# Attention, expert layer and feed-forward on one core: feed-forward tokens reordered by expert, router logits issued later

## Chip, cores and metric

The kernel runs on one core of a Trainium2 chip. The metric is device time in microseconds (us) of one execution; lower is better. The text calls the engines PE (TensorE; PEld is its weight load), DVE (VectorE), ACT (ScalarE), POOL (GpSimd) and SP (SyncE, which issues DMAs only). An engine works through its own instructions in order; semaphores order the engines among each other.

## What is computed

```python
def reference(q, k, v, proj, w_gate, w_noise, noise, w1, w2, w_in, w_out):
    # attention: 2 batches x 8 heads, 768 tokens, head size 64, masked to equal hash buckets
    mask = bucket(q @ proj)[:, :, :, None] == bucket(k @ proj)[:, :, None, :]
    x = softmax(where(mask, q @ k.T / 8, -1e9)) @ v         # as (1536 tokens, 512)
    # 8 experts, each 512 -> 1024 -> 512; the two with the largest noisy logits per token
    noisy = x @ w_gate + log1p(exp(x @ w_noise)) * noise
    top2, weight = two_largest(noisy), softmax_of_the_two
    for e in range(8):
        y[mask_e] += weight_e * (relu(x[mask_e] @ w1[e]) @ w2[e])
    # feed-forward 512 -> 2048 -> 512
    h = y @ w_in
    return (h * sigmoid(1.702 * h)) @ w_out
```

## The kernel before

Every large product is made of three passes of TensorE over 32-bit numbers that are split in a rounded ("high") part and a rest ("low" part): high x high, high x low, low x high. So each weight chunk of 128 x 1024 numbers (512 KB) passes through four hands: SP loads it into one of two buffers `staged` (`stage_chunk`, L381; chunk n is loaded only when the low part of chunk n-2 is done), ACT or POOL rounds it into the weight buffer W (`high_w` on ACT, L1292; on POOL L478), and POOL subtracts to get the low part (L480, in `split_chunk`). W holds two blocks of 8 chunks: an even and an odd one. Blocks 0 to 7 are the experts (chunks 0 to 3 are w1, 4 to 7 are w2), block 8 (`E`) is w_in, block 9 (`E + 1`) is w_out. The list `order` says in which order chunks are loaded. ACT rounds the chunks of experts 1 to 7 itself; those of blocks 0, 8 and 9 are rounded by POOL.

The stages, one after the other:

- **Attention**, to 301 us.
- **Router**, from 302 us. For each of 12 token blocks T of 128 tokens, PE transposes four pieces (L708) into one of three PSUM banks (`router_bank`), ACT takes the high part (L1256), DVE the low part (L996). After each three blocks (a group) PE computes their logits (`router_logits`, L699); ACT copies them out (L1260, L1263) and PE transposes them (L716). DVE then finds the two largest, and works out with matmuls against `one` and `tri` (L722, L723) which slot each token takes in each expert's tile of 416 rows (L1048 to L1068). Two sets of 24 small matmuls (L727, L731) turn that into the gather lists `gather_i` (L1096 and L1100).
- **Experts.** Tiles t = 0 to 7, one expert each; tiles 8 to 14 exist for experts with over 416 tokens, and none is used with these inputs. POOL gathers a tile's tokens with four indirect DMAs (`gather_x`, L521). In `expert_tile`, each of 8 steps f has PE's `hidden_up(t, f + 1)` (12 matmuls, L763) and `hidden_down(t, f)` (12 matmuls, L781), then transposes of the tile before (`transpose_y`, L794) and of the tile after (`transpose_x`, L742). ACT and DVE split the hidden values (L1285 and L1111), and the step f of tile t also has ACT's `high_w(t + 1, f)`. `rows_y` copies the finished rows and ACT sends them to `ys_dram` (L1311), with a second copy to tiles 8 to 14 (L1313), so that these hold finite numbers.
- **Feed-forward.** 12 token blocks in four groups of three. For each block POOL gathers two rows per token from `ys_dram` (`gather_y`, L579; it first waits until all rows of all used tiles have landed), ACT weights the one (`scale_x2`, L1356), DVE adds the other (`add_x2`, L1168), PE transposes (L848), and ACT and DVE split (L1360, L1172). Then in 16 steps f per group: `up(g, f + 1)` (12 matmuls, L861), sigmoid and products on ACT and DVE (L1366, L1179, L1369, L1182), `down(f)` (9 matmuls, L876). The input of the next group is made inside the steps named in `PREP = (4, 8, 12)`: scaled at f - 3, added at f - 2, transposed and split at f. A loop runs groups 0 to 2; group 3 stands alone. After each group ACT and DVE copy the outputs (L1387, L1197) and SP stores them with one DMA (L444).

## Time and profile before

| | us |
|---|---|
| median of 3 runs (lowest, highest) | 979.61 (979.21, 980.17) |
| the profiled execution | 978.34 |
| its span, first to last instruction | 976.6 |
| PE busy in the span | 884.1 (91%) |
| POOL busy | 315.0 (32%) |
| DVE, ACT busy | 402.6, 402.8 (41% each) |
| chain that ended last, PE's share | 82% |
| mean granted clock of TensorE | 0.962 of full |

Times in all rows are us from the span's start. A windows row gives, for a stretch, its length, the busy time of PE, PEld, DVE, ACT and POOL with the number of instructions, the granted clock, the DMA engines' share and GB/s.

### The profile page before, as it was taken

How to read it: one execution, taken by the hardware profiler on the slowest of the kernel's cores; microseconds unless marked ns; L12 is line 12 of the kernel's file. 1: busy time of each engine (PE TensorE's matmuls, PEld its weight loads, DVE VectorE, ACT ScalarE, POOL GpSimd, SP SyncE). 2: the span in 40 equal slices, each digit the busy share in tenths (PEclk: the TensorE clock that was granted, in tenths of full speed). 3: DMA queues.
4: the chain of work that ended last, by engine and by line, in shares of the span. 5: the costliest groups of instructions: out<-in, count | busy, mean ns of one | idle time of the engine just before them, and what ended most of it. 6: DMA issues, size and time to landing. Idle time of an engine off the chain costs nothing.

```text
span 976.6 us, 13334 instructions
## 1 busy us (share of the span) xinstructions
PE 884.1 (91%) x4910; PEld 770.6 (79%) x4910; DVE 402.6 (41%) x746; ACT 402.8 (41%) x687; POOL 315.0 (32%) x199
## 2 busy tenths in 40 slices
PE   3799999999997399999999999994699999999997
PEld 3566676676664289999999999994598999999996
DVE  4577776676864612222222222211443333333222
ACT  1566676667573223343443444411233323332222
POOL 1222020000330035655655646697971010000000
PEclk8799999999999679999999999997799999999999
DMA  7445633652323023556556555464421010000000
GB/s 164 111 116 147 168 73 95 168 125 63 93 87 109 1 74 110 190 155 184 178 159 183 166 171 173 149 200 156 140 87 44 32 43 21 32 0 0 33 1 33
DMA packets 66778, 103.34 MB, mean 106 GB/s; under 512 B 31676, under 2 KB 33724, under 8 KB 66716
## 3 DMA queue, kind: packets, MB, share of 16 engines
q1 hardware_dynamic: 55216, 76.65, 28.3%
q0 software_dynamic: 4480, 13.11, 4.5%
q10 hardware_dynamic: 7020, 12.78, 3.6%
q8 instruction: 36, 0.59, 0.2%
q14 instruction: 26, 0.21, 0.1%
HBM read 64.57 MB, written 19.07 MB: 86 GB/s over the span
## 4 chain that ended last, share of the span: by engine, by line
PE 82%; DVE 7%; ACT 3%; issue 3%; DMA 2%; SPq 2%; POOL 1%; ACTq 0%; DVEq 0%; POOLq 0%
PE psS L763 15%; PE psS L861 14%; PE psS L876 9%; PE psS L781 7%; PE psV L656 6%; PE psT L642 5%; PE psS L631 5%; PE psV L876 5%; PE psV L781 4%; PE psM L781 4%; DVE W L930 2%; PE psM L618 2%; PE psT L794 1%; ACT probT L1232 1%; PE psM L613 1%
## 5 line engine op out<-in xcount | busy, mean ns | idle before, releaser
L480 POOL TENSOR_TENSOR W<-staged,W 128x1024 fp32r<-128x1024 f32 x80 | 191.9, 2401 | 120.8 <-ACT W L1292 116.1
L763 PE MATMUL psS<-xT_hi,W 128*128 128x416 f32 x512 | 144.0, 363 | 0.8 <-DVE xT_lo L1105 0.8
L861 PE MATMUL psS<-x2T_hi,W 128*128 (+1 forms) x512 | 133.7, 342 | 1.6 <-DVE x2T_lo L1172 1.6
L1223 ACT ACTIVATE prob<-psS,exp_arg 128x768 f32<-128x768 f32 x96 | 95.5, 995 | 38.2 <-DVE exp_arg L939 38.0
L936 DVE TENSOR_REDUCE neg_max<-psS 128x1 f32<-128x768 f32 x96 | 91.5, 953 | 45.6 <-PE psS L631 44.8
L631 PE MATMUL psS<-W 128*128 128x384 f32 x384 | 93.9, 368 | 11.7 <-DMA W<-k_hi 9.6
L1232 ACT ACTIVATE probT<-psT 128x768 f32<-128x768 f32 x96 | 78.1, 813 | 57.8 <-PE psT L642 56.4
L1111 DVE SCALAR_TENSOR_TENSOR hT_lo<-psS,hT_hi 128x416 fp32r<-128x416 f32 x64 | 37.9, 592 | 152.6 <-ACT hT_hi L1285 144.2
L861 PEld LDWEIGHTS psS<-x2T_hi,W 128*128 128x128 f32 x512 | 94.2, 190 | 6.8 <-issue 2.0
L763 PEld LDWEIGHTS psS<-xT_hi,W 128*128 128x128 f32 x512 | 94.2, 191 | 2.3 <-issue 1.1
L631 PEld LDWEIGHTS psS<-W 128*128 128x128 f32 x384 | 65.1, 194 | 39.1 <-issue 34.4
L1179 DVE TENSOR_TENSOR g_sb<-psS,sig 128x384 f32<-128x384 f32 x64 | 35.7, 558 | 138.3 <-ACT sig L1366 138.3
L1366 ACT ACTIVATE sig<-psS 128x384 f32<-128x384 f32 x64 | 31.5, 492 | 144.6 <-PE psS L861 144.6
L763 PE MATMUL psS<-xT_lo,W 128*128 128x416 f32 x256 | 91.0, 355 | 0.0
L478 POOL TENSOR_TENSOR W<-staged,ones_col 128x1024 fp32r<-128x1024 f32 x24 | 45.8, 1910 | 134.8 <-DMA staged<-in_moe_w 96.3
L861 PE MATMUL psS<-x2T_lo,W 128*128 (+1 forms) x256 | 86.9, 340 | 0.0
L642 PE MATMUL psT<-ident,prob 128*128 128x128 f32 x576 | 80.7, 277 | 5.4 <-ACT probT L1232 5.3
L876 PE MATMUL psS<-W,g_hi 128*128 128x512 f32 x256 | 79.9, 393 | 2.9 <-issue 2.9
L642 PEld LDWEIGHTS psT<-ident,prob 128*128 128x128 f32 x576 | 67.3, 142 | 16.2 <-issue 12.7
L1292 ACT ACTIVATE W<-staged 128x1024 fp32r<-128x1024 f32 x56 | 59.1, 1055 | 30.7 <-DVE x_sb L1126 17.2
L781 PE MATMUL psS<-hT_hi,W 128*128 128x416 f32 x256 | 69.5, 353 | 0.0
L656 PE MATMUL psV<-probT,v_raw 128*64 128x384 f32 x360 | 68.0, 499 | 0.0
(215 smaller groups left out, 1375.5 us busy)
## 6 DMA issues: line engine op xcount, KB each, us to landing
staged<-in_moe_w SPq DMA_DIRECT2D x64, 512.0 KB
ys_dram<-x_sb ACTq DMA_DIRECT2D x60, 208.0 KB
W<-q_hi SPq DMA_DIRECT2D x32, 192.0 KB, 3.4
W<-k_hi SPq DMA_DIRECT2D x32, 192.0 KB, 3.7
staged<-in_moe_w_in SPq DMA_DIRECT2D x8, 512.0 KB
staged<-in_moe_w_out SPq DMA_DIRECT2D x8, 512.0 KB
q_raw<-in_q SPq DMA_DIRECT2D x16, 192.0 KB, 4.0
k_raw<-in_k SPq DMA_DIRECT2D x16, 192.0 KB, 3.7
```

The costliest lines, as they stand in the source:

```text
L480: nc.gpsimd.tensor_tensor(W[:, at + BLOCK:at + BLOCK + CH], staged[:, n % 2], W[:, at:at + CH].bitcast(F32), ALU.subtract).then_inc(s_spli ...
L631: last = nc.tensor.matmul(psS[:, n % 2, half, 0:HALF], stack(slot, a)[:, qt * P:(qt + 1) * P], stack(slot, b_)[:, half * HALF:(half + 1) * ...
L642: last = nc.tensor.transpose(psT[:, half, j * P:(j + 1) * P], prob[:, n % 2, c * P:(c + 1) * P], ident[:])
L656: last = nc.tensor.matmul(av_bank(hd)[half * D:(half + 1) * D, 0:HALF], v_raw[:, hd // 2 % 2, hd % 2, c * D:(c + 1) * D], probT[:, hd % 2, ...
L763: mm = nc.tensor.matmul(psS[:, 0, f % 2, 0:TM], W[:, at:at + P], x[:, t % 2, c], start=c == 0 and n == 0, stop=c == DC - 1 and n == 2)
L781: mm = nc.tensor.matmul(y_bank[d][:, 0:TM], W[:, at:at + P], h[:, f % 2], start=f == 0 and n == 0, stop=f == FC - 1 and n == 2)
L861: mm = nc.tensor.matmul(psS[:, 0, f % 2, 0:GN], W[:, at:at + P], x[:, bass.ds(buf + c * GN, GN)], start=c == 0 and n == 0, stop=c == DC - ...
L876: mm = nc.tensor.matmul(out_bank[j], gp[:, f % 2, j * P:(j + 1) * P], W[:, at:at + DM], start=f == 0 and n == 0, stop=f == GC - 1 and n == 2)
L936: nc.vector.tensor_reduce(neg_max[:, o, 0:1], psS[:, o, :, 0:HALF], mybir.AxisListType.XY, ALU.max, negate=True).then_inc(s_stat, 1)
L1223: nc.scalar.activation(prob[:, o, :].rearrange("p (a c) -> p a c", a=2), psS[:, o, :, 0:HALF], ACT.Exp, bias=exp_arg[:, o, 0:1], scale=exp ...
L1232: nc.scalar.activation(probT[:, hd % 2, :, t * P:(t + 1) * P].rearrange("p (a c) q -> p a c q", a=2), psT[:, :, 0:HALF].rearrange("p a (c ...
L1292: A(W[:, at:at + CH], staged[:, n % 2], ACT.Copy).then_inc(s_whi, 1)
```

## The change

Three parts.

1. Router: four banks instead of three; the logits of group g are issued after the transposes of group g + 1, so after blocks 5, 8 and 11, and once more at the end; ACT copies them after blocks 6, 9 and 11.
2. The order of tokens in the feed-forward. A second ranking (`mine`, `sofar`, `order_f`) sorts tokens by the larger of their two experts. Per token a record of 8 words (two slots, token number, two weights) is written to its sorted place in `rec_dram` by 12 indirect DMAs on POOL, placed ahead of the weight chunks of tile 2, behind four register loads of `needs` (how many tiles' rows each group of 384 tokens needs). SP reads the records back behind chunk (3, 7). The gathers then go by records, and the outputs are scattered to their token numbers by indirect DMAs on POOL, three per group, in place of SP's store.
3. The seam between experts and feed-forward. Group 0 is gathered, weighted and added by POOL (`first_x2`) between weight chunks, while PE is in expert 7; PE transposes it right behind expert 7 into three free banks. The chunks of w_in and w_out are loaded and split in a mixed order, w_out is rounded by ACT (`high_w(E + 1, ...)` in group 0), PE waits for halves of w_in, and `PREP` moves to (6, 10, 14). Group 0 stands outside the loop. The tiles' second copies are spread over other tiles (`filled_by`), and also go to tiles 6 and 7.

```diff
-        PREP = (4, 8, 12)
+        PREP = (6, 10, 14)
+        def filled_by(t):
+            return ((E - 2, E - 1, E), (E + 1, E + 2), (E + 3, E + 4), range(E + 5, TILES))[t] if t < 4 else ()
+        def first_bank(j):
+            return (psM, psV, psS[:, 1, 1])[j]
-        order = [(b, c) for b in range(E + 2) for c in range(8)]
+        order = [(b, c) for b in range(E) for c in range(8)]
+        order += [(E, 4), (E, 6), (E, 0), (E, 2), (E + 1, 0), (E + 1, 1), (E, 1), (E + 1, 2), (E, 3), (E, 5)]
+        order += [(E + 1, 3), (E, 7), (E + 1, 4), (E + 1, 5), (E + 1, 6), (E + 1, 7)]
...
# SP
             for block, c in order[8:8 * E]:
                 stage_chunk(block, c)
+                if (block, c) == (3, 7):
+                    sp.wait_ge(s_recs, 16 * TT)
+                    sp.dma_start(rec_s[:], rec_dram.rearrange("(t p) r -> p t r", p=P)).then_inc(s_rec, 16)
...
# POOL
-                if block in (0, E, E + 1):
+                if block in (0, E):
...
             for t in range(2, E):
                 gather_x(t)
+                if t == 2:
+                    pool.wait_ge(s_class, 1)
+                    need = [pool.value_load(needs[0:1, g:g + 1], min_val=1, max_val=TILES) for g in range(GROUPS)]
+                    for T in range(TT):
+                        nc.gpsimd.indirect_dma_start(out=rec_dram[:, :], out_offset=bass.IndirectOffsetOnAxis(ap=pos_i[:, T:T + 1].bitcast(U32), axis=0),
+                                                     in_=rec[:, T], in_offset=None).then_inc(s_recs, 16)
                 for c in range(8):
                     release(t - 2, c)
                     split_chunk(t, c)
...
             def gather_y(T):
+                j = T % GT
                 if T == 0:
-                    pool.wait_ge(s_fill, 16 * JB * (TILES - E))
-                    pool.wait_ge(s_ys, used * (16 * JB) + LEAD)
+                    pool.wait_ge(s_rec, 16)
+                    pool.wait_ge(s_fill, 16 * JB * (TILES - E + 2))
+                    pool.wait_ge(s_xT, DC * E)
+                if j == 0:
+                    pool.wait_ge(s_ys, need[T // GT] * (16 * JB) + LEAD)
...
+            def first_x2(j):
+                pool.wait_ge(s_yg[j][0], 16)
+                pool.wait_ge(s_yg[j][1], 16)
+                nc.gpsimd.tensor_tensor(yg[:, j], yg[:, j], rec_f[:, 8 * j + 3:8 * j + 5, None].to_broadcast([P, 2, DM]), ALU.mult).then_inc(s_x2a, 1)
+                pool.wait_ge(s_x2a, LEAD + j + 1)
+                nc.gpsimd.tensor_tensor(yg[:, j, 1], yg[:, j, 0], yg[:, j, 1], ALU.add).then_inc(s_x2, 1)
+            def scatter_out(g):
+                for j, (s, n) in enumerate(((s_oa, 2 * g + 1), (s_od, g + 1), (s_oa, 2 * g + 2))):
+                    pool.wait_ge(s, LEAD + n)
+                    T = GT * g + j
+                    nc.gpsimd.indirect_dma_start(out=out[:, :], out_offset=bass.IndirectOffsetOnAxis(ap=rec_s[:, T, 2:3].bitcast(U32), axis=0),
+                                                 in_=out_sb[:, j], in_offset=None).then_inc(s_out, 16)
+            split_next(E, 4)
+            split_next(E, 6)
+            for j in range(GT):
+                gather_y(j)
+            split_next(E, 0)
+            for j in range(GT):
+                first_x2(j)
+            split_next(E, 2)
+            split_next(E + 1, 0)
+            split_next(E + 1, 1)
+            for j, cs in enumerate((((E, 1), (E + 1, 2)), ((E, 3), (E, 5)), ((E + 1, 3), (E, 7)))):
+                gather_y(GT + j)
+                for bc in cs:
+                    split_next(*bc)
+            for c in range(4, 8):
+                split_next(E + 1, c)
+            for g in range(GROUPS):
+                for j in range(GT):
+                    if g + 2 < GROUPS:
+                        gather_y(GT * (g + 2) + j)
+                scatter_out(g)
...
# PE, router
-                if T >= 3:
-                    pe.wait_ge(s_rod, T - 2)
+                if T >= 4:
+                    pe.wait_ge(s_rod, T - 3)
-                if T and T % GT == 0:
+                if T >= 2 * GT - 1 and T % GT == GT - 1:
                     router_logits(T // GT - 1)
+            pe.wait_ge(s_mine, 1)
+            flat = mine[:].rearrange("p e t -> p (e t)")
+            nc.tensor.matmul(psT[:, 1, 0:TT * E], one[:], flat, start=True, stop=True)
+            nc.tensor.matmul(psT[:, 1, 256:256 + TT * E], tri[:], flat, start=True, stop=True).then_inc(s_mrank, 1)
# PE, feed-forward
                 if f % GC == 0:
+                    pe.wait_ge(s_split, split_by(E, 2))
+                if f == GC // 2:
+                    pe.wait_ge(s_split, split_by(E, 7))
...
-                    pe.wait_ge(s_split, LEAD + 8 * (E + 1) + f // 2 + 1)
+                    pe.wait_ge(s_split, split_by(E + 1, f // 2))
...
# ACT, feed-forward
+                    if first_group and f % 2 == 0 and f + 2 < GC:
+                        high_w(E + 1, f // 2 + 1)
...
+            for j in range(GT):
+                high_x2(0, j, j, True)
+            high_w(E + 1, 0)
             hidden(0, 0)
+            group(0, False, True)
```

DVE: three gate operations move from ahead of the slots' chain to its end, two (`larger`, `mine`) come ahead of it, the cast to `slot_i` goes, and sixteen small ones (the three gate operations among them) (`sofar`, `order_f`, `pos_f`, `pos_i`, `reached`, `need_f`, `needs`, `rec`) stand between the lists for the spare tiles and the cast of L1100.

## Rows read from the trace of the kernel before

**Rows 1.** Windows: an expert stretch, the seam, a feed-forward stretch.

```profile
400.00:440.00 40.00, 40.00 (x228) 39.25 (x227) 9.58 (x16) 15.94 (x25) 22.89 (x12) 1.00 0.55 168
667.60:693.50 25.90, 5.30 (x29) 3.87 (x29) 9.75 (x10) 5.97 (x10) 19.08 (x14) 0.61 0.53 164
704.00:757.00 53.00, 53.00 (x272) 47.97 (x271) 19.67 (x29) 15.80 (x30) 26.01 (x17) 1.00 0.22 74
```

**Rows 2.** Chain that ended last, in the router: start, length, what.

```profile
305.32 1.54 PE psS L699 x8
306.86 0.45 PE psT L708 x4
...
308.81 0.70 DVE xTg_lo L996
...
318.35 1.54 PE psS L699 x8
```

**Rows 3.** The same chain, end of the routing.

```profile
331.67 0.19 DVE slot_c L1065
...
341.47 4.35 PE psM L731 x24
...
346.04 0.90 issue
```

**Rows 4.** Timeline of POOL, tile 1's last chunk to tile 2's first.

```profile
395.92 1.00 POOL L521 DMA_INDIRECT x_sb<-x_dram,gather_i  x1 [0.18 <-issue]
...
399.80 0.99 POOL L521 DMA_INDIRECT x_sb<-x_dram,gather_i  x1 [0.30 <-issue]
401.63 2.38 POOL L480 TENSOR_TENSOR W<-staged,W 128x1024 fp32r<-128x1024 f32 x1 [0.84 <-PE psS L763]
```

**Rows 5.** Timeline of ACT in tile 1, step f = 2 and the next.

```profile
410.64 1.05 ACT L1292 ACTIVATE W<-staged 128x1024 fp32r<-128x1024 f32 x1
411.59 0.51 ACT L1285 ACTIVATE hT_hi<-psS 128x416 fp32r<-128x416 f32 x1
```

**Rows 6.** Chain: PE begins hidden_down(1, 4).

```profile
416.76 1.14 PE psS L781 x6
```

**Rows 7.** Timeline of SP: one load of a weight chunk issued.

```profile
638.41 0.33 SPq L381 DMA_DIRECT2D staged<-in_moe_w_in  x1
```

**Rows 8.** Timeline of POOL: that chunk waited for, and a later one rounded.

```profile
643.08 1.90 POOL L478 TENSOR_TENSOR W<-staged,ones_col 128x1024 fp32r<-128x1024 f32 x1 [0.38 <-DMA staged<-in_moe_w_in]
...
651.73 1.89 POOL L478 TENSOR_TENSOR W<-staged,ones_col 128x1024 fp32r<-128x1024 f32 x1
```

**Rows 9.** Chain across the seam between experts and feed-forward.

```profile
667.06 0.58 PE psM L781 x3
...
681.80 3.67 DMA yg<-ys_dram,slot_i
...
693.52 6.06 PE psS L861 x24
699.58 2.63 issue
...
704.57 2.11 PE psS L861 x12
```

**Rows 10.** Timeline of ACT: the last rows of tile 7 sent off.

```profile
671.72 1.00 ACTq L1311 DMA_DIRECT2D ys_dram<-x_sb  x2
```

**Rows 11.** Timeline of DVE: one low half of g, one of the next group's input.

```profile
699.18 2.73 DVE L1182 TENSOR_TENSOR g_lo<-g_sb,g_hi 128x384 fp32r<-128x384 f32 x1 [0.59 <-ACT g_hi L1369]
...
739.97 0.69 DVE L1172 TENSOR_TENSOR x2T_lo<-psT,x2T_hi 128x512 f32 x1 [1.14 <-ACT x2T_hi L1360]
```

**Rows 12.** Timeline of POOL beside the first of these.

```profile
699.16 2.35 POOL L480 TENSOR_TENSOR W<-staged,W 128x1024 fp32r<-128x1024 f32 x1
```

**Rows 13.** Chain: the transposes ahead of the second of these.

```profile
738.65 0.44 PE psT L848 x4
```

**Rows 14.** Timeline of SP: the last store.

```profile
972.94 0.33 SPq L444 DMA_DIRECT2D out<-out_sb  x1
```

More of the change, by code:

```diff
@@ L439, in _ @@
                 stage_chunk(block, c)
-            for g in range(GROUPS):
-                sp.wait_ge(s_oa, LEAD + 2 * g + 2)
-                sp.wait_ge(s_od, LEAD + g + 1)
-                half = GROUPS // B
-                sp.dma_start(out_rows[g // half, :, g % half * GT:(g % half + 1) * GT, :], out_sb[:]).then_inc(s_out, 16)
             sp.wait_ge(s_x, 16 * B)
-            sp.wait_ge(s_out, LEAD + 16 * GROUPS)
+            sp.wait_ge(s_out, 16 * TT)
         @block.gpsimd
         def _(pool):
+            nc.gpsimd.memset(rec[:].bitcast(F32), 0.0)
             nc.gpsimd.memset(ident[:], 0.0).then_inc(s_const, 1)
@@ L583, in _ @@
-            for T in range(3):
-                gather_y(T)
-            for c in range(1, 8):
-                release(E - 1, c)
-                split_chunk(E + 1, c)
-                if c % 2 and 3 + c // 2 < 6:
-                    gather_y(3 + c // 2)
-            for T in range(6, TT):
-                gather_y(T)
+                    nc.gpsimd.indirect_dma_start(out=yg[:, j, k_], out_offset=None, in_=ys_dram[:, :],
+                                                 in_offset=bass.IndirectOffsetOnAxis(ap=rec_s[:, T, k_:k_ + 1].bitcast(U32), axis=0)
+                                                 ).then_inc(s_yg[j][k_], 16)
```

167 lines of the change are left out of this document (102 added, 65 removed).

## The prediction

> **What bounds the kernel now.** I read the page first, then windows by stage, then the chain of waits at each place that the change touches. In an expert stretch PE is busy for all of the 40 us at the full clock, and POOL for 22.9; in the first feed-forward group PE is again full, 53 of 53 us, with POOL at 26.0 [rows 1]. In these stages time is lost only if somebody makes PE wait. The seam between them is different: 25.9 us with 5.3 us of PE work at a mean clock of 0.61 [rows 1]. The chain there runs from PE's last matmul (ends 667.64) over the landing of tile 7's rows, the gathers and the first weighted blocks to PE's first `up` at 693.52 [rows 9]. The router is a second place: its logits come every 4.34 us (three periods from 305.32 to 318.35), while the PE work in a period is 1.57 + 3 x 0.45 = 2.9; PE waits for DVE's low halves [rows 2]. ACT, DVE and POOL are at or under 41% elsewhere, but their order matters: each is a queue, and PE's next operand may stand behind a wait of another's.
>
> **Router.** Four banks and later logits let transposes 3 to 5 run before the first logits, which can still start at 305.3. From there PE has 1.54 + 1.35 per group. The last logits then need the twelfth low half; at the pace of 0.6 to 0.7 us a piece [rows 2], behind ACT, I get 313.1 in place of 318.35: **-5.2** (PE's work alone would give 312.7, -5.6; if ACT's copies delay the last pieces, -4.5). The sixteen small DVE operations at about 0.2 us [rows 3], a few of them 0.3, make some 3.8 us. They run beside 24 matmuls of 4.35 us, after which comes the cast that PE waits for: nothing; without that cover up to 1. The two operations ahead of the slots take the place of three.
>
> **Tile 1: POOL comes late.** Before, POOL issues the last gather for tile 2 at 399.80 and takes the low part of chunk (2, 0) at 401.63, without a pause [rows 4]. Now four register loads and twelve indirect DMAs stand between. Each DMA costs a pitch of 1.29 (395.92 to 399.80 are three) [rows 4]; that is for gathers of 104 rows, and scatters of 32 bytes a row are not in this trace. Twelve make 15.2. For a register load the nearest row is PE's: 0.90 us from `gather_i` to its first matmul [rows 3], of which 0.14 is the usual gap, so 0.76 each, 3.0 together. So POOL is free at 400.8 + 3.0 + 15.2 = 419.0, and (2, 0) is split at 421.5. Only then may SP load chunk (2, 2). A load that was waited for took 643.08 - 638.41 = 4.67 [rows 7, 8], so it lands at 426.2. ACT has that rounding as its work at 410.64 [rows 5] and is an in-order queue: behind it stands the rounding of hT for `hidden_down(1, 4)`. 1.05 + 0.51 on ACT, 0.59 on DVE and gaps put it at 428.6, where PE began at 416.76 [rows 6]: 11.8 lost. After it each second chunk has a cycle of load 4.67, rounding 1.05, low part 2.38 and gaps, 8.4 us, against 9 to 10 of PE, so the queue recovers slowly; working it through gives two more waits of 1.0 and 1.4, and PE restarts at the lower clock (1.2 GHz; 24 matmuls took 6.06 in place of 2 x 2.11 [rows 9]), of which about 0.5 is not covered by these. **+14.5.** Lower bound 0: if the block took under 6.1 us, the rounding would come within the 3.4 us of slack that hT has (`down` and `up` of 2.3 each, less 1.2 for ACT and DVE). Upper bound +18, at 1.3 us per load and 1.4 per DMA. ACT's extra copies of tile 0's rows (two more issues per step) fit in that slack: nothing, at most 1. SP's reading of the records sits behind chunk (3, 7), whose follower is wanted 9 us later: nothing, at most 3.
>
> **Seam.** POOL has done (7, 7) at 633.9. Then: four splits of w_in at 4.3, the step that rows 8 show twice over (643.08 to 651.73), six gathers at 1.26, and three times a multiply of 1.9 and an add of half of 2.4: 17.3 + 7.6 + 9.6 = 34.5, so 668.4. Bounds for `first_x2`, which the trace doesn't show: 2.6 to 6 us each; the ends are 667 and 677. PE has group 0's transposes done at 671.9. ACT is bound by the sending of tile 7's rows to 672.72 [rows 10]; three roundings at a pitch of 0.5 and a DVE low half of 0.69 bring PE's first `up` to 675.2 in place of 693.52: **-18.3**. Before, the first `down` came 8.7 us behind it: slow clock 1.84, and a `g_lo` of 2.73 us where others take 0.56. That one is put down as 2.63 of "issue" [rows 9], but it ran from 699.18 beside a POOL subtract of 699.16 to 701.51 and ended 0.4 behind it [rows 11, 12]. With POOL idle there it is 4.6; PE pauses for only 3.3 us now, and whether the clock falls in that, as it did in the 25.9 us (mean 0.61 [rows 1]), no row decides; I take half: **-3.2** (-4.1 or -2.3).
>
> **Group 0: POOL is the bound.** PE could start `up(0, 8)` at 675.2 + 8 x 2.11 + 7 x 2.10 + 0.8 = 707.5. It needs (E, 7). POOL can't start on (E + 1, 1) before ACT has rounded it, behind `hidden(0, 1)`: 682.2. Then in its queue: low part 2.4, two gathers 2.5, split 4.3, 2.4, 2.5, two splits 8.7, 2.5, 2.4, split 4.3, and gaps: 715. So 7.2 lost, of which PE stands 5 at `down(6)`. To this comes what rows 11 and 12 show: DVE's SBUF-with-SBUF subtract is held to the end of a POOL operation, then holds POOL for 0.4. Six such meetings in POOL's chain add 2.5: **+9.7** (5 to 13). The Trainium skill ("SBUF — State Buffer", section "SBUF: two separate sides") says that DVE and GpSimd take one shared pair of ports as an exclusive lock for a whole instruction; the trace agrees (2.73 for 0.56), and by it `hidden`'s other operations, with PSUM on one side, stay untouched, as do those of expert 7.
>
> **PREP (6, 10, 14).** The last block of the next group is now transposed at f = 14, and the next thing that PE does is `up(g + 1, 0)`, which needs its low half. That came at 740.66, 1.57 behind PE's transposes (738.65 + 0.44) [rows 11, 13]. Before, one more step covered it. Three group changes at 1.6: **+4.8** (3.9 to 5.4).
>
> **Tail.** SP's one store, issued at 972.94 [rows 14], becomes three scatters, the first from 972.5, the third from 975.1. Landing 3.67 behind its issue, as a gather [rows 9], it ends at 978.7 against 976.6: **+2.1** (0.5 to 4). By the Trainium skill ("DMA: Bandwidth & Descriptors", section "Anatomy of one DMA — SWDGE (gpsimd) path"), 2.0 us and 0.6 for 256 KB, this term would be 1.1, an estimate; the rows are longer, and I go by them.
>
> **Sum.** -5.2 - 18.3 - 3.2 + 14.5 + 9.7 + 4.8 + 2.1 = +4.4. The profiled execution has 978.34 for a span of 976.6 and would have 982.7. It lies 1.3 under the median of 979.61, so I forecast **984.0**.
>
> **Rivals.**
> 1. *POOL's record writes are cheap.* If a 32-byte scatter costs about what a direct DMA costs ACT (0.3 to 0.5 us) and the loads little, the block stays at or near 6 us and PE doesn't stop in tile 1: 984.0 - 14.5 = 969.5, faster. It decides at 6.1 us for the whole block; at 12 us the time would be 976. For it: the data are small. Against: the issue of a gather looks like a fixed cost. Chance 0.2.
> 2. *They are dearer.* The same block at 25 to 30 us, because twelve in a row wait for room: 994. For it: PE then also meets the low clock twice. Against: six gathers in a row kept their pitch. Chance 0.1.
> 3. *The first group isn't ready at the seam.* `first_x2` at 6 us each or gathers later than I have them put (E, 2) behind 675.2, by 2 to 5 us: 988. POOL was busy all through expert 7 already. Chance 0.1.
> 4. *Group 0 isn't starved*: ACT and POOL interleave better than my chain, 5 us less: 979, no change. Chance 0.1.
>
> **Numbers.** Forecast as worked out 0.5, own range 978 to 990. About 0.2% (2 us) is what a measurement can tell from no change. Slower by more: 0.5 x 0.75 + 0.1 + 0.1 + a little of the fourth = 0.58. Faster by more: rival 1's 0.2, a share of the others, 0.26. Within: 0.16. The range takes in most of rivals 1 and 2: 971 to 993.
>
> **What the profile would show.** Right: a PE gap of some 12 us in tile 1 with ACT's L1292 waiting for a load; logits 2.9 us apart; the first `up` about 8 us behind the last `down` of tile 7; PE waiting at f = 6 and 8 of group 0 for POOL's low parts; three waits of 1.6 at the group changes. Wrong: POOL done with its record writes before about 407; no wait at f = 8; a seam over 12 us.

## The result and the profile after

The changed kernel takes **990.25 us** (median of 4 runs, 989.34 to 991.05) against 979.89 for the kernel before (4 runs, 979.21 to 981.80): ratio 1.0102, 95% interval 1.0084 to 1.0121. That is 1.0% slower, in the direction of the forecast of 984.0 and inside its range of 971 to 993, though just outside the 978 to 990 of the case that was worked out; it is slower by 10.4 us where 4.4 were forecast. The profiled execution has 991.04 for a span of 989.3; the one before had 978.34 for 976.6. So 12.7 us of span have to be explained.

Windows of the kernel after: the expert stretch of [rows 1], the seam, the first feed-forward group, the other three; then a short one behind a group change. The columns are those of [rows 1].

```profile
400.00:440.00 40.00, 34.61 (x169) 31.23 (x168) 8.21 (x14) 13.34 (x20) 26.21 (x17) 0.87 0.49 151
673.30:685.20 11.90, 3.83 (x28) 3.23 (x28) 4.34 (x7) 4.62 (x8) 1.15 (x1) 0.84 0.39 121
685.20:763.40 78.20, 70.57 (x340) 62.72 (x340) 30.66 (x38) 26.41 (x45) 49.11 (x28) 0.96 0.31 102
763.40:978.00 214.60, 210.59 (x1041) 189.50 (x1041) 63.62 (x111) 59.29 (x114) 14.58 (x16) 0.98 0.06 21
836.00:838.00 2.00, 2.00 (x7) 1.90 (x7) 0.00 (x0) 0.43 (x1) 0.00 (x0) 0.50 0.00 0
```

The seam shrank from 25.9 to 12.0 us, as meant. But PE, which was busy for all of 40 us in tile 1, now stands for 5.4 of them, and the feed-forward got longer throughout.

The chain that ended last in the kernel after. L835 and L853 are the experts' up and down (before L763, L781), L868 the transposes of their rows, L967 the new transposes of group 0, L938 and L953 the feed-forward's up and down (before L861, L876), L922 the next group's transposes, L1457 their high half on ACT.

```profile
404.58 0.93 issue
405.51 0.35 PE psS L835
...
672.68 0.58 PE psM L853 x3
...
676.40 4.02 issue
680.42 0.63 PE psM L967 x4
...
684.20 1.03 issue
685.24 5.81 PE psS L938 x24
...
831.77 0.45 PE psT L922 x4
...
832.34 0.61 ACT x2T_hi L1457
832.95 1.13 issue
834.08 3.46 PE psS L938 x12
```

In tile 1 there are gaps of about 1 us between single matmuls, from 404.58 to 412.37, that nothing in the profile explains. At 676.40 there are 4 us in which PE waits for nothing that the profile shows; before, PE had nothing to do there anyway. At 832 is the pause at a group change, and behind it twelve matmuls take 3.46 us in place of 2.11: the granted clock had fallen.

Timeline of POOL in the kernel after: the end of tile 2's gathers (L552), twelve record scatters (L575), the low parts (L510); group 0's splits; the last output scatter.

```profile
394.98 0.98 POOL L552 DMA_INDIRECT x_sb<-x_dram,gather_i  x1 [0.30 <-issue]
396.27 1.02 POOL L575 DMA_INDIRECT rec_dram<-rec,pos_i  x1 [0.31 <-issue]
...
410.22 0.96 POOL L575 DMA_INDIRECT rec_dram<-rec,pos_i  x1 [0.30 <-issue]
411.21 4.67 POOL L510 TENSOR_TENSOR W<-staged,W 128x1024 fp32r<-128x1024 f32 x2
...
662.40 1.29 POOL L630 TENSOR_TENSOR yg<-yg 128x512 f32<-128x512 f32 x1
...
685.30 2.38 POOL L510 TENSOR_TENSOR W<-staged,W 128x1024 fp32r<-128x1024 f32 x1 [10.86 <-ACT W L1389]
693.82 2.40 POOL L510 TENSOR_TENSOR W<-staged,W 128x1024 fp32r<-128x1024 f32 x1 [6.14 <-ACT W L1389]
...
720.03 2.35 POOL L510 TENSOR_TENSOR W<-staged,W 128x1024 fp32r<-128x1024 f32 x1
722.33 1.90 POOL L505 TENSOR_TENSOR W<-staged,ones_col 128x1024 fp32r<-128x1024 f32 x1
...
981.46 0.96 POOL L636 DMA_INDIRECT out<-out_sb,rec_s  x1 [0.30 <-issue]
```

Four things are read here. From the last gather to the first scatter it is 1.29, the ordinary pitch, so the four register loads between them cost nothing. The twelve scatters have a mean pitch of 1.27 (eleven from 396.27 to 410.22), close to a gather's 1.29 [rows 4]. Between 674.4 and 693.8 POOL stands idle for 17 us, waiting for ACT to round two chunks of w_out, and is then the engine that PE waits for. And the splits in group 0 meet DVE's work; the timeline of DVE shows a `g_lo` of 4.41 us, which ends 0.4 behind the second of the POOL operations of 720.03 and 722.33:

```profile
720.24 4.41 DVE L1281 TENSOR_TENSOR g_lo<-g_sb,g_hi 128x384 fp32r<-128x384 f32 x1 [0.59 <-ACT g_hi L1466]
```

PE's waits within group 0 (us in total, times, longest) name POOL:

```profile
PE psS L953 <- POOL W L510: 5.1, 1, 5.1
```

### The profile page after: what moved, and what is told of

It reads as the page before. It is cut to its first block, busy times and chain, and to the rows that moved or that the text cites. A ratio compares the mean times of both kernels' runs of the same rounds, so it can differ in the third digit from the quotient of the medians.

```text
span 989.3 us, 13343 instructions
## 1 busy us (share of the span) xinstructions
PE 892.9 (90%) x4912; PEld 776.0 (78%) x4912; DVE 404.9 (41%) x757; ACT 409.1 (41%) x692; POOL 332.0 (34%) x223
## 4 chain that ended last, share of the span: by engine, by line
PE 78%; DVE 7%; issue 5%; POOL 4%; ACT 2%; SPq 2%; DMA 1%; POOLq 0%; ACTq 0%; DVEq 0%
PE psS L835 15%; PE psS L938 13%; PE psS L953 8%; PE psS L853 7%; PE psV L724 6%; PE psS L699 5%; PE psT L710 5%; PE psV L953 4%; PE psV L853 4%; PE psM L853 3%; DVE W L1009 2%; POOL W L510 2%; PE psM L686 2%; PE psT L868 1%; PE psM L681 1%
## 5 line engine op out<-in xcount | busy, mean ns | idle before, releaser
L510 POOL TENSOR_TENSOR W<-staged,W 128x1024 fp32r<-128x1024 f32 x80 | 192.0, 2402 | 151.5 <-ACT W L1389 127.9
L835 PE MATMUL psS<-xT_hi,W 128*128 128x416 f32 x512 | 145.3, 364 | 4.1 <-issue 3.3
L938 PE MATMUL psS<-x2T_hi,W 128*128 (+1 forms) x512 | 135.3, 346 | 8.5 <-issue 8.3
L938 PEld LDWEIGHTS psS<-x2T_hi,W 128*128 128x128 f32 x512 | 95.4, 193 | 14.6 <-issue 6.1
L835 PEld LDWEIGHTS psS<-xT_hi,W 128*128 128x128 f32 x512 | 94.5, 192 | 7.0 <-issue 5.8
L835 PE MATMUL psS<-xT_lo,W 128*128 128x416 f32 x256 | 91.5, 357 | 2.0 <-issue 2.0
L938 PE MATMUL psS<-x2T_lo,W 128*128 (+1 forms) x256 | 88.2, 344 | 0.0
L1389 ACT ACTIVATE W<-staged 128x1024 fp32r<-128x1024 f32 x64 | 67.5, 1055 | 47.4 <-issue 23.2
L953 PE MATMUL psS<-W,g_hi 128*128 128x512 f32 x256 | 81.5, 400 | 6.0 <-POOL W L510 5.1
L505 POOL TENSOR_TENSOR W<-staged,ones_col 128x1024 fp32r<-128x1024 f32 x16 | 30.7, 1918 | 135.2 <-DMA staged<-in_moe_w 97.0
L853 PE MATMUL psS<-hT_hi,W 128*128 128x416 f32 x256 | 70.3, 356 | 0.1
```

Of the source, the lines that this page charges most:

```text
L510: nc.gpsimd.tensor_tensor(W[:, at + BLOCK:at + BLOCK + CH], staged[:, n % 2], W[:, at:at + CH].bitcast(F32), ALU.subtract).then_inc(s_spli ...
L835: mm = nc.tensor.matmul(psS[:, 0, f % 2, 0:TM], W[:, at:at + P], x[:, t % 2, c], start=c == 0 and n == 0, stop=c == DC - 1 and n == 2)
L853: mm = nc.tensor.matmul(y_bank[d][:, 0:TM], W[:, at:at + P], h[:, f % 2], start=f == 0 and n == 0, stop=f == FC - 1 and n == 2)
L938: mm = nc.tensor.matmul(psS[:, 0, f % 2, 0:GN], W[:, at:at + P], x[:, bass.ds(buf + c * GN, GN)], start=c == 0 and n == 0, stop=c == DC - ...
L953: mm = nc.tensor.matmul(out_bank[j], gp[:, f % 2, j * P:(j + 1) * P], W[:, at:at + DM], start=f == 0 and n == 0, stop=f == GC - 1 and n == 2)
L1389: A(W[:, at:at + CH], staged[:, n % 2], ACT.Copy).then_inc(s_whi if block <= E else s_ohigh, 1)
```

## Experiments

Milestones of each profiled execution (e3 is told in its own place), in us: end of the last `down` of tile 7, start of the first `up` of group 0, end of the last matmul, end of the span. They are read from the chain and PE's timeline. The stages between them can be compared across chips. Each kernel but e8 and e9 ran once, and single totals differ by a few us: nine runs of the kernel before on one chip lie between 977.06 and 982.90. A part of that is the end of attention, which the change leaves alone: the router's first transposes begin at 301.99 (before), 303.24 (after), 302.00 (e1), 304.09 (e5). It shifts the first two columns.

| kernel | last down | first up | last matmul | end | up to last matmul | tail |
|---|---|---|---|---|---|---|
| before | 667.64 | 693.52 | 971.80 | 976.6 | 278.3 | 4.8 |
| after | 673.26 | 685.24 | 978.04 | 989.3 | 292.8 | 11.3 |
| e1 | 671.72 | 684.38 | 969.33 | 980.6 | 285.0 | 11.3 |
| e2 | 662.43 | 696.79 | 990.90 | 1001.3 | 294.1 | 10.4 |
| e4 | 672.92 | 685.37 | 976.68 | 981.8 | 291.3 | 5.1 |
| e5 | 663.94 | 674.57 | 967.71 | 979.0 | 293.1 | 11.3 |
| e6 | 671.79 | 679.30 | 969.52 | 980.8 | 290.2 | 11.3 |
| e7 | 671.38 | 684.10 | 965.02 | 976.3 | 280.9 | 11.3 |
| e8 | 664.06 | 678.65 | 955.02 | 966.3 | 276.4 | 11.3 |
| e9 | 662.67 | 670.23 | 946.11 | 957.3 | 275.9 | 11.2 |
| e10 | 671.33 | 682.88 | 974.44 | 985.7 | 291.6 | 11.3 |
| e11 | 673.05 | 685.61 | 979.71 | 990.9 | 294.1 | 11.2 |
| e12 | 672.26 | 684.48 | 978.68 | 988.2 | 294.2 | 9.5 |

The first four ran on one chip beside one run of the kernel before (977.69).

**e1: the group change.** The next group's input goes back to one step before the end.

```diff
-        PREP = (6, 10, 14)
+        PREP = (6, 10, 13)
```

> The changed kernel with PREP = (6, 10, 13) in place of (6, 10, 14): one step of 4.2 us stands between the last transposes of the next group's input and the up that needs them. Theory A (each pause of 1.9 us at a group change also sends TensorE to its lower clock at the two later changes, 3.46 and 3.90 us for 12 matmuls in place of 2.11): from the start of group 1 to the last matmul 207 us in place of 214.7, and 2 us at the first change, about 9.5 in all, so 981. Theory B (only the pauses cost, the slow matmuls have another cause, for instance the scatters): 5.5 less, 985, and slow matmuls behind the changes stay.

982.33 us, nearer to A, and by A's mechanism. The pauses at the group changes are gone, and at the same place in e1 the clock stays full:

```profile
836.00:838.00 2.00, 2.00 (x12) 1.83 (x11) 0.11 (x1) 0.75 (x2) 1.65 (x2) 1.00 0.21 86
```

From group 1's first `up` to the last matmul e1 takes 207.1 us (from 762.28), the kernel after 214.7 (from 763.37); with the first pause the placement costs the profiled execution 9.5 us. (First up to last matmul fell by only 7.8, from 292.8 to 285.0, because e1's group 0 took 1.6 longer without its pause, 0.7 of it in the first 24 matmuls: 6.52 against 5.81.) The pause itself is 1.86 (832.22 to 834.08) and the twelve matmuls behind it take at least 2.37 in place of 2.11: 2.1 each, 6.4 for three. The other 3.1 are the lower clock that followed the second and third pause (3.46 and 3.90 for the twelve, and slow matmuls in the `down` behind them). The same pauses are in e4, e6 and e7, there with 2.36 to 2.38 each time; in e2, e3, e5, e10, e11 and e12 it is 3.15 to 3.86 after the second and third, and never so after the first. What decides between the two no run shows.

**e2: one direct write of the records.** The scatters and the register loads go; the records lie in token order, so the tokens are not sorted, and the gathers of every group wait for all tiles.

```diff
-                    need = [pool.value_load(needs[0:1, g:g + 1], min_val=1, max_val=TILES) for g in range(GROUPS)]
-                    for T in range(TT):
-                        nc.gpsimd.indirect_dma_start(out=rec_dram[:, :], ..., in_=rec[:, T], in_offset=None).then_inc(s_recs, 16)
+                    need = [used] * GROUPS
+                    nc.gpsimd.dma_start(rec_dram.rearrange("(t p) r -> p t r", p=P), rec[:]).then_inc(s_recs, 16 * TT)
```

> The changed kernel without the record scatters: the records are written by one direct DMA from POOL's queue, in token order, and every group waits for all used tiles (the sorting is left out, the output is unchanged). Tile 1 is what is read. Theory A (the twelve scatters starve PE and ACT of instructions, 404 to 413 us) and theory B (POOL's block makes the load of chunk (2, 2) late) both expect no stop in tile 1: last down of tile 7 about 4.3 us ahead of the kernel before, at 663.3, 9.9 ahead of the changed one. If neither holds (the extra copies of tile 0's rows by ACT are the cause), the stop of about 9 us stays. The seam gets longer, since group 0 can't be gathered before tile 7 is stored.

1003.0 us, but tile 1 runs without a stop: PE is busy for 8.00 of 8.00 us in 406 to 414, and the last `down` ends at 662.43 in place of 673.26. This kernel still has ACT's extra copies of tile 0's rows, so these are not the cause of the stop. What is lost is the seam: 34.4 us, since the first group now waits for tile 7's rows and everything behind them hangs on POOL. This is the other side of the change: the sorting by expert is what makes the early gathers possible, and it is worth over 20 us at the seam.

**e3: gathers in place of the scatters.** Twelve indirect gathers of the same 32-byte records, behind the direct write, whose landing they wait for. SP's reading of the records goes too.

```diff
-                    need = [pool.value_load(needs[0:1, g:g + 1], min_val=1, max_val=TILES) for g in range(GROUPS)]
+                    need = [used] * GROUPS
+                    nc.gpsimd.dma_start(rec_dram.rearrange("(t p) r -> p t r", p=P), rec[:]).then_inc(s_recs, 16 * TT)
+                    pool.wait_ge(s_recs, 16 * TT)
                     for T in range(TT):
-                        nc.gpsimd.indirect_dma_start(out=rec_dram[:, :], ..., in_=rec[:, T], in_offset=None).then_inc(s_recs, 16)
+                        nc.gpsimd.indirect_dma_start(out=rec_s[:, T], out_offset=None, in_=rec_dram[:, :], ...).then_inc(s_rec, 16)
```

> As the one before, but twelve indirect gathers of 32-byte records, from DRAM, stand at the scatters' place, with the same pitch on POOL (no sorting; the output is unchanged). Theory A (it is the scattered writes that starve the engines): no matmul gaps of 1 us with nothing awaited inside one up; the stop then is that of the late load of chunk (2, 2), with ACT's rounding waiting for the load, about 7 to 9 us at down(1, 4). Theory B (any indirect DMA in a row does it): the same gaps as with the scatters.

1021.34 us; the last `down` ends at 680.15 and the seam is 34.4, as in e2. The twelve gathers run from 403.92 to 418.70, a pitch of 1.26: direction and row size don't matter to the issue. The block ends 7.6 us later than with the scatters (411.1), and PE's `hidden_down(1, 4)` begins at 426.75 in place of 419.12 (e1), 7.6 later too. The delay of POOL goes one to one into PE, and no single matmuls 1 us apart are seen. The chain in e1 shows the path link by link, the same as the forecast's: the last low part, SP's load of (2, 2), ACT's rounding, `hT` behind it in ACT's queue, DVE, PE.

```profile
411.09 2.37 POOL W L510
...
413.48 3.38 DMA staged<-in_moe_w
...
417.85 0.51 ACT hT_hi L1382
...
418.38 0.60 DVE hT_lo L1210
...
419.12 2.42 PE psS L853 x6
```

**e4: the last store by SP.** The last 384 tokens' rows are stored by one plain DMA of SP, so they stay in sorted order.

```diff
+        s_last = sem("s_last")
...
-            sp.wait_ge(s_out, 16 * TT)
+            sp.wait_ge(s_out, 16 * (TT - GT))
+            sp.wait_ge(s_oa, LEAD + 2 * GROUPS)
+            sp.wait_ge(s_od, LEAD + GROUPS)
+            sp.dma_start(out.rearrange("(t p) d -> p t d", p=P)[:, TT - GT:TT], out_sb[:]).then_inc(s_last, 16)
+            sp.wait_ge(s_last, 16)
...
-                scatter_out(g)
+                if g + 1 < GROUPS:
+                    scatter_out(g)
```

> The changed kernel with the last group stored by one direct DMA of SP (after the other groups' scatters have landed), so that the last 384 rows are not brought to their tokens' places. Theory A (the landing of a scatter into DRAM takes some 7.5 us from its issue, 11.3 us from the last matmul to the end): the end comes 4.8 us behind the last matmul, 6.5 less in all, 984. Theory B (the end of the program itself costs more with the changed kernel): 11 us stay.

983.57 us; the tail is 5.1 in place of 11.3, so the scatters cost 6.2 there, three times the forecast term.

The next four ran on another chip (before: 980.37, median of 9 runs, 977.06 to 982.90).

**e5: the record scatters spread.** One behind each of the first twelve splits of tiles 2 and 3.

```diff
-                    for T in range(TT):
-                        nc.gpsimd.indirect_dma_start(out=rec_dram[:, :], ...).then_inc(s_recs, 16)
                 for c in range(8):
                     release(t - 2, c)
                     split_chunk(t, c)
+                    T = 8 * (t - 2) + c
+                    if T < TT:
+                        nc.gpsimd.indirect_dma_start(out=rec_dram[:, :], ...).then_inc(s_recs, 16)
```

> The twelve record scatters no longer stand in one block ahead of tile 2's chunks but one behind each of the first twelve chunk splits (tiles 2 and 3). Theory A (the block as such makes POOL late by 15 us, so that chunk (2, 2) is loaded late and ACT's wait for it holds the hidden values of step 4): a scatter of 1.3 us fits into each split's slack (POOL is busy 22.9 of 40 us), PE does not stop in tile 1, its last down of tile 7 ends 5 to 6 us earlier, and the time is 990.3 - 6 to -10 = 980 to 984. Theory B (what delays tile 1 is the code of the added instructions or the records' traffic, wherever they stand): PE still loses 5 us or more in tiles 1 to 3, and the time stays at 988 to 991.

980.72 us. The last `down` of tile 7 ends at 663.94 in place of 673.26, though attention ended later here. So it is measured from the 24 matmuls behind the routing lists (L731 before, L803 in the kernel after, at 337.15; at 337.99 in e5): to the last `down` it is 326.0 us here, 326.2 in the kernel before, 326.0 to 326.1 in e2, e8 and e9. In the eight profiles that have the block it is 335.3 to 336.1. The stop in tile 1 is gone; the block as such was the cause, it costs 9 to 10 us, and the same twelve DMAs cost nothing in the splits' slack.

**e6: no code for tiles 8 to 14.** The branches around this code, whose body is never entered with these inputs (each engine jumps over it), are left out on all engines: such a kernel can't handle an expert with over 416 tokens.

```diff
# SP
-            stage_over(E, used)
# POOL, PE, DVE and ACT
-            over(E)
```

> The branches for tiles 8 to 14 (never taken with these inputs) are left out on all engines; nothing else changes. At the seam the chain has 4.0 us of issue ahead of PE's first transposes of group 0 (2.9 in another execution), for which nothing that the profile shows is waited for. Theory A (the engine is jumping over the untaken code, whose length it has to skip and refetch): these 4.0 us shrink to under 1, and the time falls by 3 to 4 us, to about 986 to 987. Theory B (the gap is the fixed cost of the first instructions behind the register-dependent wait, or of the gathered rows' arrival that the profile puts down as issue): it stays at 3 to 4 us, and the time is 989 to 991.

982.86 us, 3 to 4 better than A: the clock held at the group changes here, which is worth 3.0. Behind the transposes of tile 7's rows the chain has no gap on PE any more; it now runs over DVE's and ACT's copies of these rows, as the forecast had it, and the first `up` comes 7.5 us behind the last `down` (forecast 675.2 - 667.6 = 7.6):

```profile
673.01 1.07 PE psT L866 x8
674.10 0.70 DVE x_sb L1222
...
677.17 1.09 ACT x2T_hi L1452 x2
678.26 1.03 issue
679.30 6.00 PE psS L935 x24
```

So passing the unused code costs PE the 4.0 us (2.3 to 5.3 in the other profiles with it and a short seam). The kernel before has the same branches; that their cost lay hidden there in the 25.9 us of waiting is inferred, since its profile shows no such gap.

**e7: another order of the weights.** (E, 1) and (E, 3) come ahead of (E + 1, 0), in the load list and in POOL's queue, where POOL stood idle.

```diff
-        order += [(E, 4), (E, 6), (E, 0), (E, 2), (E + 1, 0), (E + 1, 1), (E, 1), (E + 1, 2), (E, 3), (E, 5)]
+        order += [(E, 4), (E, 6), (E, 0), (E, 2), (E, 1), (E, 3), (E + 1, 0), (E + 1, 1), (E, 5), (E + 1, 2)]
...
-            for j, cs in enumerate((((E, 1), (E + 1, 2)), ((E, 3), (E, 5)), ((E + 1, 3), (E, 7)))):
+            for j, cs in enumerate((((E, 5), (E + 1, 2)), ((E + 1, 3), (E, 7)), ())):
```

> Only the order of the chunks of w_in and w_out changes: (E, 1) and (E, 3) come ahead of (E + 1, 0), so that POOL splits them while it now idles from 674 to 685 waiting for ACT's first rounding of w_out. Theory A (POOL's queue, idle 10.9 us there and late afterwards, is what starves group 0): PE's wait of 5.1 us at step 6 goes, group 0's length from the first up to group 1's falls from 78.1 to 71 to 74, and the time is 984 to 987. Theory B (group 0 is held by the DVE low halves that meet POOL operations, wherever POOL's order puts them): group 0 shrinks by under 2 us, and the time is 988 to 991; the waits move to (E + 1, 0) and (E + 1, 1), which now come later.

978.02 us, better than either theory had it (the clock also held at the group changes, 3.0, and attention ended 1.2 earlier). From the first `up` to group 1's first it is 69.3 us in place of 78.1. POOL's timeline shows the splits of (E, 1) and (E, 3) in the former idle time, and POOL then waits only 0.94 us for ACT's rounding of (E + 1, 0):

```profile
672.70 1.90 POOL L505 TENSOR_TENSOR W<-staged,ones_col 128x1024 fp32r<-128x1024 f32 x1
...
679.12 1.89 POOL L505 TENSOR_TENSOR W<-staged,ones_col 128x1024 fp32r<-128x1024 f32 x1 [2.10 <-DMA staged<-in_moe_w_in]
...
684.39 2.40 POOL L510 TENSOR_TENSOR W<-staged,W 128x1024 fp32r<-128x1024 f32 x1 [0.94 <-ACT W L1391]
```

PE's wait of 5.1 us for POOL is gone and no other has come. So group 0 was starved by POOL's queue. DVE's collisions with POOL go on (POOL's pair of low parts at 698.15 takes 5.10, nominally 4.7), but nobody waits for what they delay. The gain of 8.8 is more than the wait of 5.1, because the clock had fallen twice in the kernel after: at the start (24 matmuls in 5.81, here 4.45) and behind the wait (0.57 from 722 to 726, where the nine matmuls of `down` and a transpose took some 1.5 longer). The first of these doesn't belong to the order: e10 below has the old order, a wait of 5.2 for POOL and as fast a start (4.48), and takes 76.9 us to group 1's first `up`. So the order is worth 7.6.

**e8: PREP, spread and order together.**

> Three changes together: PREP = (6, 10, 13), the record scatters spread over tiles 2 and 3, and the weight order of the run before this. If the three causes are separate and add up (theory A): 990.3 - 8.5 (PREP) - 6 to 10 (spread) - 4 to 6 (order) = 966 to 972, faster than the kernel before by 0.8 to 1.4%. If they overlap, because what one frees the next wait takes up (theory B): no better than 976, within 0.4% of the kernel before.

964.1 us (5 runs, 962.18 to 968.02), ratio to the kernel before 0.9829 (0.9808 to 0.9851): the three repairs add up, better than A's 966 to 972, which had priced the order at 4 to 6; the change is then worth 1.7%. Last `down` 664.06, first up to last matmul 276.4. The seam is still 14.6 us in this profile, the longest of the five executions; the chain has 3.53 of issue on PE and 3.79 on ACT.

The last four ran beside 7 runs of the kernel before (979.92).

**e9: e8 without the branches of e6.**

> The combined version (964.1 us median) without the branches for tiles 8 to 14, which these inputs never take. Theory A (PE and ACT each lose time in skipping that code at the seam, 3.53 and 3.79 us of issue in the combined version's chain, and nothing is late behind it): both gaps go and the time is 964.1 - 6 to -7.5 = 956.5 to 958. Theory B (POOL's queue, which the faster seam now meets earlier, takes part of it back as waits in group 0): 959 to 962.

959.48 us (4 runs, 958.33 to 960.58), ratio 0.9793 (0.9771 to 0.9816). Both gaps are gone (seam 7.6) and group 0 gives nothing back (275.9 against 276.4), so B's mechanism is not seen, though the time lies in B's 959 to 962. The gain between the medians is 4.6, less than A's 6 to 7.5, which was read from e8's profiled execution, the longest of its five (968.02). It is an upper bound of what a cheaper way past the branches would bring, not a version to use: it lacks part of the kernel's generality.

**e10: one branch in place of seven nested ones.** The recursion ends at tile 8.

```diff
-                if t == TILES:
+                if t == E + 1:
```

> The changed kernel with one spare tile's branch (tile 8) in place of seven nested ones; it is still not taken. Theory A (the cost of skipping a branch is one refetch at its target, whatever the length): the gap ahead of PE's first transposes of group 0 stays at 2.7 to 4 us, the first up comes 11 to 12 us behind the last down, as in the changed kernel. Theory B (the cost goes with the length of the skipped code): the gap shrinks to under 1 us, the seam is 7.5 to 8.5 us, as without any branch.

987.42 us, the seam 11.6. The gap on PE is as long as with all seven tiles' code:

```profile
674.47 4.15 issue
678.62 1.09 PE psM L967 x4
```

The cost goes with there being a jump, not with the length skipped. The DMA queues that load instructions point to what it is: between 664 and 686 us they carry, in the kernel after (packets, MB, share of 16 engines),

```profile
q8 instruction: 2, 0.03, 0.6%
q14 instruction: 4, 0.03, 0.4%
```

and without the branches (e6)

```profile
q8 instruction: 1, 0.02, 0.3%
q14 instruction: 2, 0.02, 0.3%
```

That is twice the packets in the same stretch; e10 has 3 and 2, and the kernel before has 2 and 4, as the kernel after. In windows of 1 us q8's two packets are at 677 and 680 in the kernel after, whose gap is 676.40 to 680.42, and two of e10's at 675 and 678, whose gap is 674.47 to 678.62; e6 has none on q8 from 664 to 681. The Trainium skill ("Runtime: NRT & Kernel Launch", section "Instruction fetch mechanics") says that engines fetch their code ahead in sequence, and that a taken branch to a place not yet held must first load the block at its target. By that rule one tile's code costs as much as seven, as soon as it is longer than what is held; the trace agrees (4.15 and 4.02). No row joins a packet to the stalled engine or tells how much is held, and no run moved the target's code, so the link itself is not shown.

**e11: narrow output scatters.** 512 bytes a row instead of 2 KB, in all groups; three quarters of the output are left out.

```diff
-                    nc.gpsimd.indirect_dma_start(out=out[:, :], ..., in_=out_sb[:, j], in_offset=None).then_inc(s_out, 16)
+                    nc.gpsimd.indirect_dma_start(out=out.rearrange("t (a n) -> (t a) n", a=4), ..., in_=out_sb[:, j, 0:DM // 4], in_offset=None).then_inc(s_out, 16)
```

> Every output scatter carries 128 columns (512 bytes a row) in place of 512 (2 KB a row); three quarters of the output are left out. Behind the last matmul the changed kernel has 11.3 us, of which 7.8 from the issue of the last scatter. Theory A (the size of the data sets the landing): the end comes 2 us or more earlier, 9.3 us or less behind the last matmul. Theory B (a fixed cost of the scatter's completion): within 1 us of 11.3.

992.7 us; the tail is 11.2. The size of the data doesn't count.

**e12: plain stores on POOL's queue.** The last group's three stores go to consecutive rows, so these rows stay in sorted order.

```diff
+                    if g == GROUPS - 1:
+                        nc.gpsimd.dma_start(out[T * P:(T + 1) * P, :], out_sb[:, j]).then_inc(s_out, 16)
+                        continue
```

> The last group's three stores stay on POOL's queue, but as plain DMAs to consecutive rows, not scatters by index; the last 384 tokens' rows are so left in sorted order. With SP's one plain store the end came 5.1 us behind the last matmul, with POOL's scatters 11.3. Theory A (POOL's queue itself, with its descriptors written by software, makes the landing late): the end stays 9.5 to 11.5 us behind the last matmul. Theory B (the indexed rows do it, 128 of them gathered from the index list): 5 to 7.5 us.

989.91 us, tail 9.5, at the lower edge of A. Windows over the tail show where it goes. The kernel after (last column but one: the share of the DMA engines):

```profile
981.80:983.30 1.50, 0.00 (x0) 0.00 (x0) 0.00 (x0) 0.00 (x0) 0.62 (x1) 0.50 0.57 232
983.30:984.80 1.50, 0.00 (x0) 0.00 (x0) 0.00 (x0) 0.00 (x0) 0.00 (x0) 0.50 0.22 90
984.80:986.30 1.50, 0.00 (x0) 0.00 (x0) 0.00 (x0) 0.00 (x0) 0.00 (x0) 0.50 0.00 0
```

e12, plain stores by POOL (span ends at 988.2):

```profile
982.20:983.70 1.50, 0.00 (x0) 0.00 (x0) 0.00 (x0) 0.00 (x0) 0.00 (x0) 0.68 0.45 180
983.70:985.20 1.50, 0.00 (x0) 0.00 (x0) 0.00 (x0) 0.00 (x0) 0.00 (x0) 0.50 0.00 0
```

e4, SP's store (span ends at 981.8):

```profile
980.30:981.80 1.50, 0.00 (x0) 0.00 (x0) 0.00 (x0) 0.00 (x0) 0.00 (x0) 0.76 0.35 132
```

With SP the span ends in the window in which the last data move. With POOL's queue, scattered or plain, no data move for the last 4.5 us at least. Finer slices put the last bytes at 983.7 in the kernel after and at 983.0 in e12, 5.6 and 5.2 before the end; with SP at 980.9 in e4 and at 975.7 in the kernel before, 0.9 before the end. This difference of 4.3 to 4.7 us is the larger part of the 6.5; the indexed form adds 1.8 (its three issues take 3.49 us, 978.93 to 982.42, the plain ones 1.70). What the queue does in the 5 us no row shows.

## Why the prediction was off

By its own terms, forecast against the span of the profiled execution:

| term | forecast | measured | difference |
|---|---|---|---|
| end of attention | 0 | +1.3 | +1.3 |
| router | -5.2 | -5.6 | -0.4 |
| tile 1 | +14.5 | +9.9 | -4.6 |
| seam | -18.3 | -13.9 | +4.4 |
| group 0 (-3.2 + 9.7) | +6.5 | +5.0 | -1.5 |
| group changes | +4.8 | +9.5 | +4.7 |
| tail | +2.1 | +6.5 | +4.4 |
| sum | +4.4 | +12.7 | +8.3 |

Seam, group changes and tail are the steps that failed, by 4.4 to 4.7 each; tile 1 was oversized by as much. The end of attention is no effect of the change that any run shows: it lies at the time of the kernel before in e1 and e7. (Seam and tail are differences of the milestones, group 0 ends at group 1's start with the first pause taken off, and the group changes are 214.66 - 207.06 for the last three groups plus that pause; attention, router and tile 1 are the three parts of the last `down`'s shift of +5.6.)

**Router: right.** The 24 matmuls behind the lists came 4.3 us earlier, at 337.15 in place of 341.47 [rows 3], though the router's first transposes began 1.25 later. Chain before, then after:

```profile
301.99 0.64 PE psT L708 x4
```

```profile
303.24 0.64 PE psT L776 x4
...
337.15 4.34 PE psM L803 x24
```

So the router itself gained 5.6 (39.48 us from the one to the other before, 33.91 after; 33.9 in e1, e5 and e7 too). The sixteen small operations took DVE from 337.01 to 341.38, beside 24 matmuls from 337.15 to 341.49, and the cast that PE waits for began at 341.53: the cover held, as forecast.

**Tile 1: right mechanism, two sizes wrong.** The path from POOL over SP's load to ACT's queue is what e1's chain shows, and e5 shows that the block's place is the cause. The block was forecast at 3.0 + 15.2 and took 14.9: "for a register load the nearest row is PE's: 0.76 each" failed, the four were free. And the load that was waited for took 3.38, not 4.67. A shift of POOL's end goes one to one into PE (e3). Counted from the matmuls behind the lists, e1's `hidden_down(1, 4)` came 7.9 later than before (83.2 against 75.3), forecast 11.8. Behind it the lower clock cost 1.9 in that `down` and the transposes, and no further wait came; forecast were two waits of 1.0 and 1.4 and 0.5 for the clock (with the 11.8 these make 14.7, not 14.5).

The profiled execution of the kernel after stopped in another way, at the same price. Its matmuls of one `up` came singly, with gaps of 0.9 to 1.1 us, from 404.6 to 412.4, and the clock was 0.50 from 410 to 418. ACT stood too: its `hT_hi`, whose `up` had ended at 401.30, came at 414.03, 9.05 us behind ACT's operation before it. When the late chunk was rounded (timeline of ACT), PE hadn't come to the `down` behind it (chain), so it didn't wait for it:

```profile
417.19 1.05 ACT L1389 ACTIVATE W<-staged 128x1024 fp32r<-128x1024 f32 x1
```

```profile
422.38 1.14 PE psS L853 x6
```

From the matmuls behind the lists to the last `down` it took 336.1 us, the seven other profiles with the block 335.3 to 336.0, so the gaps took the place of the late load's wait and added at most 0.8. The gaps end with POOL's block, but none of the other profiles with the same code has them; their cause is open.

**Seam: one missing term.** With the branches gone (e6) it is 7.5 us against the forecast's 7.6, so each step of that sum was right, and POOL's `first_x2` was fast enough (1.90 + 1.29 a block, bounds 2.6 to 6). What the sum lacked was the time in which PE, and in some executions ACT, get past the unused code. "PE has group 0's transposes done at 671.9" assumed that they follow at once. Before, this time was hidden, as inferred at e6, by the waiting that the change removed. No row of before priced it, but the place should have got a bound: PE's next instruction stands behind a branch.

**Group 0: right, 1.5 too much.** PE stood 5.1 us at `down` 6, as the working had it, for POOL. e7 shows the cause as forecast: POOL couldn't start on w_out before ACT, and stood 17 us idle. The -3.2 and the +9.7 can't be parted in the profile; the sum was +5.0. No wait of note came at `up(0, 8)` (0.18), since the one at `down` 6 had covered it: of the forecast's own signs of being wrong this one came.

**Group changes: the wait nearly right, the clock left out.** From group 1's first `up` e6, with full clock, needs 4.5 us more than e1 (211.6 against 207.1), and 1.9 for the first pause: 6.4, forecast 4.8. "Three group changes at 1.6" priced the wait at full clock behind it. The profile puts the rest together: a pause is 1.86 and its re-start 0.26 rather than 1.6, together those 6.4 for three (+1.6), and the clock, which fell after two of the three (0.50 in 836 to 838). From group 1's first `up` to the last matmul it was 214.66 us against 211.61 in e6, which has the pauses and not the fall: +3.0. 1.6 + 3.0 is the missing 4.6. The forecast had charged slow matmuls after the long stops but not after these short ones.

**Tail: wrong row.** "Landing 3.67 behind its issue, as a gather" took an incoming gather, released when its data had come, as the measure for a store at the program's end. It was 7.8 (981.46 to 989.3). By the figures of the Trainium skill ("DMA: Bandwidth & Descriptors", section "Anatomy of one DMA — SWDGE (gpsimd) path"), a fixed part and one that grows with the bytes, the whole term would have been 1.1, an estimate. No run here supports it: the landing alone is 7.8, and in e11, with a quarter of the bytes, it is 7.8 too (983.13 to 990.9). No row of before shows a store from POOL's queue, so the upper end ought to have been wider than 4.

**Rivals.** The first (cheap record writes) is refuted by the pitch of 1.27, though half of its reason held: the loads are free. The second (dearer) and the third (group 0 not ready: POOL's last block was ready at 670.14, ahead of PE) didn't occur. The fourth (group 0 not starved) is refuted by the 5.1 us. The truth was no rival but the forecast's case with three terms larger; that tile 1 was too large by 4.6 made the sum look better than its parts.

## What to carry to other kernels

When a change takes away a long wait, ask what else happened inside that wait: a branch passed, a queue drained. It was free and will now be on the path. Work that an in-order engine has slack for must be dealt out over that slack: twelve DMAs in a block cost 9 to 10 us, between the splits nothing; and a queue that idles while it waits for another engine should be given the chunks that it can do alone (7.6 us here). A last store belonged on SP's queue here (6.2 us), where its form allows it, and an operand needed at a loop's edge should be ready one step earlier, since a pause of 1.9 us can bring slow matmuls behind it.

## What the runs showed of the hardware

- An indirect DMA takes POOL 1.25 to 1.29 us to issue whether it gathers or scatters and whether a row has 32 bytes, 512 bytes or 2 KB (e3, e11 and the kernel after). A plain one took 0.57 (e12) and 1.14 (e2).
- A DMA from POOL's queue at the program's end: the span ends 5.2 to 5.6 us after the last bytes moved (e12, the kernel after), against 0.9 for SP's (e4, the kernel before).
- Jumping over unused code cost PE 2.3 to 5.3 us, the same for one tile's code as for seven, and on ACT up to 3.8 more.
- A `g_lo` of 0.56 us on DVE took 4.41 beside two POOL operations in a row. The rule that the forecast cited on the shared pair of ports (the Trainium skill, "SBUF — State Buffer", section "SBUF: two separate sides") fits: the `g_sb` operations of the same group, with PSUM on one side, kept 0.56 beside POOL's subtracts (at 704.91, beside the pair of 700.61).
- Behind a pause of 1.9 us at a group change TensorE's granted clock fell to half, its lower level of 1.2 GHz, in seven profiles (after, e2, e3, e5, e10, e11, e12) and stayed full in three (e4, e6, e7) with the same code at that place; never behind the first of the three pauses.
- In one profile PE's matmuls in tile 1 came singly, with gaps of 0.9 to 1.1 us that nothing in the profile explains; no other profile of the same code has them.
